# Four small moves in the queues of a fused attention and feed-forward kernel: three match products, the order of two transposes banks, and the softmax sums

## The reference

```python
# q, k, v: 2 batches x 8 heads x 768 tokens x 64; proj: 64 x 6
q_bits = (q @ proj > 0);  k_bits = (k @ proj > 0)
q_bucket = sum(q_bits * 2**arange(6));  k_bucket = sum(k_bits * 2**arange(6))
scores = q @ k.T / sqrt(64)
scores = where(q_bucket[:, None] == k_bucket[None, :], scores, -1e9)
attn = exp(scores - max(scores))
attn = attn / (sum(attn) + 1e-9)
out = attn @ v
```

## Time and profile before

| | us |
|---|---|
| median of 3 runs | 493.43 (493.28 to 494.02) |
| the profiled execution | 493.24 |
| its span, first to last instruction | 491.3 |
| PE busy | 476.4 (97%) |
| DVE busy | 350.3 (71%) |
| ACT busy | 283.8 (58%) |
| POOL busy | 254.7 (52%) |

### The profile page before, as it was taken

One profiled execution on the slowest core, in us unless ns is written; L12 is line 12 of the kernel. 1 busy time (PEld: TensorE's weight loads), 2 busy tenths in 40 slices (PEclk: granted clock), 3 DMA queues, 4 the chain that ended last, 5 costly groups with the idle time before them and its releaser, 6 DMA issues.

```text
span 491.3 us, 9460 instructions
## 1 busy us (share of the span) xinstructions
PE 476.4 (97%) x3541; PEld 404.1 (82%) x3541; DVE 350.3 (71%) x611; ACT 283.8 (58%) x601; POOL 254.7 (52%) x250
## 2 busy tenths in 40 slices
PE   8889999999999999999999999999999999999997
PEld 6666766766766766776769998999999999999997
DVE  5878787988979879786687987785687498226211
ACT  5887878777877887876645433452443354244130
POOL 5853718456391753724177637465466358246140
PEclk9999999999999999999999999999999999999999
DMA  6300310303012030200220001001001000100101
GB/s 227 119 1 18 102 49 2 134 18 132 19 45 93 17 133 17 70 18 17 87 86 1 3 1 43 1 1 45 2 1 33 12 1 3 43 1 3 42 2 43
DMA packets 10557, 20.69 MB, mean 42 GB/s; under 512 B 1680, under 2 KB 6928, under 8 KB 10512
## 3 DMA queue, kind: packets, MB, share of 16 engines
q1 hardware_dynamic: 10224, 19.94, 11.9%
q10 hardware_dynamic: 288, 0.15, 0.1%
HBM read 16.94 MB, written 3.15 MB: 41 GB/s over the span
## 4 chain that ended last, share of the span: by engine, by line
PE 78%; DVE 11%; ACT 5%; issue 5%; POOL 1%; DVEq 0%; POOLq 0%; ACTq 0%
PE ps L667 28%; PE ps L675 12%; PE ps L620 12%; PE ps L655 11%; PE ps L631 11%; DVE gate L850 2%; ACT probs L427 2%; PE ps L641 2%; PE ps L594 1%; PE ps L685 1%; DVE tmp_a L925 1%; ACT q L419 1%; DVE negmax L807 1%; DVE tmp_b L923 1%; DVE pt L814 1%
## 5 line engine op out<-in xcount | busy, mean ns | idle before, releaser
L807 DVE TENSOR_REDUCE negmax<-ps 128x1 f32<-128x768 f32 x96 | 91.7, 956 | 25.7 <-PE ps L620 22.9
L427 ACT ACTIVATE probs<-ps,negmax 128x768 f32<-128x768 f32 x96 | 86.6, 902 | 15.8 <-DVE negmax L807 13.5
L620 PE MATMUL ps<-k,q 128*128 128x384 f32 x384 | 92.1, 361 | 3.5 <-ACT probs L427 3.4
L631 PE MATMUL ps<-ident,probs 128*128 128x128 f32 x576 | 81.8, 275 | 3.5 <-DVE pt L814 3.1
L631 PEld LDWEIGHTS ps<-ident,probs 128*128 128x128 f32 x576 | 66.2, 140 | 14.3 <-DVE pt L814 5.0
L620 PEld LDWEIGHTS ps<-k,q 128*128 128x128 f32 x384 | 63.1, 189 | 11.8 <-ACT probs L427 11.2
L655 PE MATMUL ps<-pt,vals 128*64 128x384 f32 x384 | 68.8, 494 | 1.3 <-ACT pt L435 0.6
L384 POOL TENSOR_TENSOR h_lo<-tmp_b,h_hi 128x256 fp32r<-128x256 f32 x48 | 38.7, 811 | 45.9 <-ACT h_hi L534 45.9
L435 ACT ACTIVATE pt<-ps 128x384 f32<-128x384 f32 x96 | 46.8, 488 | 16.2 <-PE ps L631 15.4
L814 DVE COPY pt<-ps 128x384 f32<-128x384 f32 x96 | 52.1, 543 | 3.6 <-PE ps L631 3.6
L850 DVE SCALAR_TENSOR_TENSOR gate<-x,conv_sb,gate 128x256 f32<-128x256 f32 x96 | 52.8, 550 | 2.2
(11 more groups left out here) (86 smaller groups left out, 1161.3 us busy)
## 6 DMA issues: line engine op xcount, KB each, us to landing
w_raw<-w SPq DMA_DIRECT2D x8, 640.0 KB, 4.3
raw_q<-qT SPq DMA_DIRECT2D x8, 384.0 KB, 5.3
raw_k<-kT SPq DMA_DIRECT2D x8, 384.0 KB, 4.7
vals<-v SPq DMA_DIRECT2D x16, 192.0 KB, 2.4
out<-w_raw SPq DMA_DIRECT2D x24, 128.0 KB, 1.7
w_raw<-w SPq DMA_DIRECT2D x4, 512.0 KB, 3.3
codes_b<-codes ACTq DMA_DIRECT2D x1, 128.0 KB, 4.2
proj_bd<-proj ACTq DMA_DIRECT2D x1, 16.0 KB, 3.3
```

Source lines behind the costliest of these rows:

```text
L427: act.activation(probs[par][:, :], score[par], ACT.Exp, bias=negmax[:, t:t + 1], accum_out=sums[:, t, 0:1]).then_inc(exp_done, 1)
L620: last = pe.matmul(ps[:, 2 * par + half, 0:HALF], qq[h][:, q], kk[h][:, half * HALF:(half + 1) * HALF], start=first, stop=not first)
L631: last = pe.transpose(tbank[u][:, k * P:(k + 1) * P], probs[g % 2][:, kt * P:(kt + 1) * P], ident[:, :])
L807: dve.tensor_reduce(negmax[:, t:t + 1], score[g % 2], AX.XY, ALU.max, negate=True).then_inc(max_done, 1)
```

## The change

Three edits, all in the order of the queues. Matches 1, 2 and 3 move to t = 1, 4 and 7, behind the transposes. In the step after a `spread`, `transposes` fills bank 5 first and bank 4 second (and `exp_tile`, which must know that both have read its buffer, waits for the one that is now last). `add_eps` and `reciprocals` of the head before move on DVE from the first step of a head (t = 0 and 6, around `tile_max`) to its third (t = 2 and 8, behind `tile_max`, ahead of `second_half_up`).

```diff
-MATCH_AHEAD, MATCH_BEHIND = {2: 1, 5: 2}, {5: 3}
+MATCH_STEPS = {1: 1, 4: 2, 7: 3}
...
+def after_spread(g):
+    return g >= KT and g % KT == R_STEP + 1
...
             def exp_tile(g):
                 par, t = g % 2, g % TILES
                 act.wait_ge(max_done, g + 1)
-                wait(act, tr_done[1], g - 1)
+                if g >= 2 and after_spread(g - 2):
+                    act.wait_ge(tr_done[0], turns0((g - 2) // KT, (g - 2) % KT) + 1)
+                else:
+                    wait(act, tr_done[1], g - 1)
...
             def transposes(g):
-                for u in range(2):
+                for u in (1, 0) if after_spread(g) else (0, 1):
...
-                if 0 < i < LAST and t in MATCH_AHEAD:
-                    match(i + 1, MATCH_AHEAD[t])
+                if 0 < i < LAST and t in MATCH_STEPS:
+                    match(i + 1, MATCH_STEPS[t])
                 if tt in PV_STEPS and head:
                     product(head - 1, PV_STEPS[tt])
                 if tt == R_STEP and head:
                     spread(head - 1)
                 if t == TILES - 1 and i + 2 < PAIRS:
                     match(i + 2, 0)
-                if 0 < i < LAST and t in MATCH_BEHIND:
-                    match(i + 1, MATCH_BEHIND[t])
...
-                if tt == 0 and head:
-                    add_eps(head - 1)
                 if t == R_STEP and i:
                     normalise(head - 2)
                 if g + 2 < PAIRS * TILES:
                     tile_max(g + 2)
-                if tt == 0 and head:
+                if tt == R_STEP and head:
+                    add_eps(head - 1)
                     reciprocals(head - 1)
                 second_half_up(g)
```

## The result

The changed kernel takes 498.68 us (median of 5 runs, 498.51 to 499.16), the kernel before 493.28 beside it; the ratio is 1.0106, with a 95% interval of 1.0093 to 1.012. It is slower by 5.4 us, where 4.3 were forecast (497.7, range 494.4 to 499.5). The profiled execution took 498.68 us with a span of 496.6.

A forecast was written before the change was run, and what follows sets the result against it. PE, 97% busy, was taken to be bound by attention-stage waits. Pairs 2 to 4 add 2.19 us, 1 and 6 1.42, 5 0.65, 0 and 7 0.05: +4.3, so 497.7 us, range 494.4 to 499.5.

The forecast's parts named there:

- What bounds the kernel: Attention stage: in steps without a product PE waits on the scores, maximum, exponential loop; weight loads waited 5.6 us.
- Match 2 leaves t = 5: Pairs 1 to 6: product and all behind it 0.17 us earlier; the match costs 0 in t = 4.
- add_eps and reciprocals leave t = 0 and 6: DVE, pairs 1 to 6: 0.20 us gained at t = 6 and 0.05 at t = 0, for scores(10).
- They arrive in t = 8, and POOL slips between the taps: Taps pushed 0.30 us on DVE; POOL's L302 comes 0.32 behind the first tap and goes ahead of the second.
- the pairs with a margin of 0.06: Pairs 1 and 6: second tap starts 0.38 behind the first, POOL at 0.32, still ahead; price 0.71 us.
- The price: Pairs 2 to 4: tile_max(11) 5.07 after tile_max(10) instead of 3.92, 1.15 later, less 0.42 gained: +0.73 us each.
- Bank 5 first: Step after a spread: ACT's bank 4 copy about 0.2 us later, exponential some 0.08 later, covered by the collision in pairs 1 to 6.
- POOL's slack: Second widening on POOL ends at 121.53, spread needs it at 121.84: 0.3 us of slack, cost taken as 0.
- No collision: Rival, chance 0.14: taps and POOL keep clear, pairs 1 to 6 gain 0.34 us each, 491.5 us.
- Collision in pairs 2 to 4 alone: Rival, chance 0.13: pairs 1, 5 and 6 escape on margins of 0.06 to 0.08; +1.2 us, 494.6.
- the cover go: Rival, chance 0.06: collision plus matches unhidden in t = 1 and 7, or late widening; up to 499.5 us.
- the price half of mine: Rival, chance 0.03: ACT or PE has more slack, price per collision halves and the edits cancel within 0.2%.

The follow-up runs named there:

- pushing the taps alone: Kernel before with two tensor_reduces put behind tile_max(10) on DVE, ahead of the taps at t = 8; 500.49 us, ratio 1.0143.
- POOL held: Changed kernel with one wait added on POOL: low_queries(2i+3) waits until the second tap of t = 8 is done; 491.88 us, ratio 0.9969.
- the two kernels in which the collision is taken away: Changed kernel with low_queries on POOL waiting for the second tap of t = 8, 491.88 us; changed kernel with hot_keys behind the taps, 492.05 us.
- the best order of the queues: Changed kernel with POOL's low_queries waiting for the second tap of t = 8 and bank 4 first everywhere; 490.55 us, ratio 0.9941.
- the two with memsets: Kernel before with one or four DVE memsets of one column put ahead of the two taps at t = 8; 490.93 and 490.76 us.
- the two of the last runs: Kernel before, tiles from the gate on 64 bytes further: 496.91 us; changed kernel with POOL's wait and bank 4 first, 32 bytes further: 487.86 us.

## Why the prediction was right

**What bounds the kernel.** Right. The stalls of PE in the steps without a product are where gains and losses arose, and the matrix stage was only shifted: 236.64 us from its first y matmul to the end before (254.66 to 491.3), 236.66 after (259.94 to 496.6).

**Match 2 leaves t = 5, at 0.17.** Right: 0.9 us for the matches alone, against 1.0. Match 1 is hidden, as taken; match 3 all but: with the matches alone the scores of t = 8 are 3.52 us behind those of t = 6, and 3.49 before.

**add_eps and reciprocals leave t = 0 and 6.** Right. From the scores of t = 0 to those of t = 8 are 17.86 us before (100.75 to 118.61), 17.62 with the sums and reciprocals moved alone (103.05 to 120.67), 0.24 less against 0.25, and 17.46 in the changed kernel (102.63 to 120.09), 0.40 less against 0.42 with the match. The 0.20 stands at t = 7, as said; the other 0.04 stands at t = 2, where I had put 0.05 at t = 0.

**They arrive in t = 8, and POOL slips between the taps.** Right, and shown: taking POOL's turn away alone removes 6.8 us, and pushing the taps alone creates 7.0 us. POOL enters where the sum had it, 0.15 ahead of the first tap's recorded end (124.11 + 1.93 - 1.84 = 124.20, against 123.87 + 0.48 = 124.35), and the two taps take the 2.45 us that were worked out. It happened in all six pairs (tile_max(11) at 5.18, 5.28, 5.27, 5.26, 5.13 and 5.18 behind tile_max(10)); the pairs with a margin of 0.06 were not an exception, and had 0.14, since the push was larger than I had it. The taps of pair 1 (a first tap, then one with two inputs) in the changed kernel:

```profile
63.51 0.34 DVE L854 TENSOR_SCALAR gate<-x,conv_sb 128x256 f32<-128x256 f32 x1
63.89 1.98 DVE L857 SCALAR_TENSOR_TENSOR gate<-x,conv_sb,gate 128x256 f32<-128x256 f32 x1
```

"A tap with two inputs in SBUF" was too narrow a name for what POOL holds up. In pair 5 the held tap is the first tap of a sum, a TENSOR_SCALAR with one large input, and it is held like the others. It takes 1.92 us here and 0.34 with POOL held. DVE, then POOL, of the changed kernel:

```profile
184.32 0.47 DVE L857 SCALAR_TENSOR_TENSOR gate<-x,conv_sb,gate 128x256 f32<-128x256 f32 x1
184.71 1.92 DVE L854 TENSOR_SCALAR gate<-x,conv_sb 128x256 f32<-128x256 f32 x1
```

```profile
184.56 1.94 POOL L308 TENSOR_TENSOR q<-raw_q,q 64x768 fp32r<-64x768 f32 x1 [0.54 <-ACT q L457]
```

**The price, where the step was mis-sized.** In pairs 2 to 4 I had tile_max(11) at 5.07 behind tile_max(10); it is 5.27. Two terms of the sum were wrong, for one reason: the spacing of neighbours on DVE. "Each pair of them pushes what is behind it on DVE by 0.20 + 0.10 = 0.30": the copy came 1.30 behind tile_max in place of 0.88, so 0.42, because add_eps does not start 0.08 before tile_max ends, as the copy did, but 0.03 behind its end. The earlier trace rows show both, add_eps 0.03 behind the end of normalise and the copy 0.08 ahead of the end of reciprocals, and I used the second spacing for the first. The copy gave back 0.04 of it, so the taps moved by 0.38 (2.78 behind tile_max(10) where they were 2.40). And the DVE instruction behind a held tap starts 0.04 after its end, not 0.08 before: 0.12 more. Together 0.38 - 0.30 + 0.12 = 0.20 a pair. In pairs 1, 5 and 6, where I had taken off 0.02 to 0.08, it is 0.13 or 0.14. All six make 1.0 us, which is the difference between +4.3 and the +5.3 of the spans.

**Bank 5 first.** Right in its sign, too small by half: "by some 0.08" was 0.17. In the kernel before, the exponential at 124.55 stood both 0.05 behind the end of tile_max and 0.03 behind the end of the copy, with no overlap; I took it to have 0.12 us of room on the copy's side. In the changed kernel the collision covers this in pairs 1 to 6, as said: in pair 3 the exponential of t = 9 waits 1.18 us for DVE's maximum, with the copy long done.

**POOL's slack.** Right: the spread follows the scores of t = 8 by 3.63 us (120.09 to 123.72) and did by 3.65 before; the widening ended at 123.56, 0.16 ahead of it. Half of the 0.3 that I had counted was gone, because the first widening stands at 6.40 us in the pair (102.63 to 109.03) and not at 6.25 (100.75 to 107.0). From there to the second one are 14.03 us, as worked out. The waits of the changed kernel name POOL as what the weight loads of the spread waited for, 12 times 0.6 us, but they stood idle for the same 0.6 before, so this is not a delay.

**The rivals.** "No collision" was worked out at 491.5; the two kernels in which the collision is taken away stand at 491.9 and 492.1, and the difference is the bank order's other 0.09 a pair. "Collision in pairs 2 to 4 alone" did not occur, nor did the cover go, nor was the price half of mine.

## What to carry to other kernels

Before adding work to a queue with idle time behind it, look not only at who waits for that queue but at who shares something with it. Two instructions on different engines that hang from the same event keep their distance from it (POOL's 3.02 us, the same in every kernel here that puts no wait on it), and a push of a quarter of a microsecond on one side can exchange their order. The sign of such a case in a trace is an instruction that lasts longer than its like (here 2.06 us for a POOL operation of 1.84). It shows that the two already touch; how far they are from the other order is read from their starts (here 0.62 against 0.51). And when an engine's busy time grows while it has the same instructions (DVE, 10.9 us), look for waiting that is recorded inside them. Here one wait that fixes the order was worth 6.8 us, more than any of the moves: with it, and without the exchange of the banks, the change is a gain of 0.6%. What it is that the two engines share, no run here shows.

## What the runs showed that I had not expected

Where the tiles lie in SBUF changes the pace of the matmuls in the matrix stage, with PE's clock at full in all cases. In the kernel before, the moving operands of the matrix stage start 32 bytes past a multiple of 128 (x_hi at byte 121248). From one matmul of L667 to the next are 0.117 us there, 0.115 on the mean with everything behind neg_two 32 bytes further, and 0.120 with 64 bytes further; the matmuls of L675, with both operands moved alike, stayed at 0.120. The matrix stage takes 236.6, 234.2 and 240.2 us at these three placements. That it is the placement of the moving operand against the weights of w1, which did not move, is a guess; no run here separates it.

So 32 unused bytes were worth 2.7 us (490.55 to 487.86), nearly as much as the whole of the best order of the queues, 2.9. A kernel that gains or loses half a percent when a tile is added or widened should be compared at equal placement. All kernels here but the two with memsets and the two of the last runs have the placement of the kernel before.

The other surprise is in the memsets: four of them on DVE moved the tap by 0.03 us (2.43 behind tile_max(10) in place of 2.40).
